# Another order of filler matmuls, search steps and low parts in the routing of a three-stage kernel

## Chip, core and metric

The kernel runs as one program on one core of a Trainium2 chip. A core has five engines with queues of their own: PE (TensorE, matmul), DVE (VectorE), ACT (ScalarE), POOL (GpSimd) and SP, which here only issues DMAs. They run at the same time and wait for each other by semaphores. The metric is the device time of one execution in microseconds (us).

## What is computed

Three stages, one behind the other, all in float32: a linear attention with a decaying state, a dense feed-forward layer, and a layer of 8 experts in which each expert gets exactly 3072 / 8 = 384 rows. Who gets which row is settled in order of the logits: the largest one first, and an expert that is full takes no more.

```python
def _attn_ref(r, k, v, w, u):                  # r, k, v: (4, 8, 768, 48)
    for t in range(S):
        cur = np.einsum('bhd,bhe->bhde', u[None] * kt, vt)
        y[:, :, t] = np.einsum('bhd,bhde->bhe', rt, state + cur)
        state = w[None, :, :, None] * state + np.einsum('bhd,bhe->bhde', kt, vt)

def _moe_ref(x, w_in, w_out, alpha):           # 3072 x 384, 384 x 2048, 2048 x 384
    h = x @ w_in
    g = np.maximum(h, 0.0) + alpha * np.minimum(h, 0.0)
    return g @ w_out

def _moe2_ref(x, w_gate, w1, w2):              # 8 experts, 384 x 1024 and 1024 x 384
    order = np.argsort(-(x @ w_gate).flatten())
    for idx in order:
        tok, e = (int(idx) // E, int(idx) % E)
        if assigned[tok] >= 0 or counts[e] >= cap:
            continue
        assigned[tok] = e
        counts[e] += 1
    for e in range(E):
        mask = assigned == e
        out[mask] = np.maximum(x[mask] @ w1[e], 0.0) @ w2[e]
```

## The kernel before

**Precision.** A float32 product is made of three matmuls of a faster type. Each operand is split in a high part (a copy made on ACT, the names end in `h`) and a low part (the difference, made on DVE or POOL, the names end in `l`), and `product3` adds high x high, high x low and low x high (L1410 to L1412).

**Stages.** Up to about 513 us the kernel computes attention and the first feed-forward layer in six chunks of rows. Then come eight routing rounds and eight experts, overlapped: while PE works for one expert, the search for a later one runs on DVE and PE.

**A routing round** (`route(p)`, L1345) finds which expert fills up next and its 384 rows. It is a search for the value of a logit, in six steps (two levels of three). Step m: DVE compares all keys with 40 marks (`grid`, L1296 or L1298); PE counts the hits for each expert (`count(p, m)`, 12 small matmuls, L1677); DVE turns the counts into hits (`rest`, `hits`, L1303 and L1304); PE adds up which mark was met (`digit(p, m)`, one small matmul, L1712); DVE takes the maximum, the answer (`found`, L1307), and makes the next grid from it. Then `close` (L1309) works out the expert number (`expert`, L1317) and a running sum, PE adds offsets over partitions (`offsets`, L1716), DVE makes slots, `inversion` turns them into matrices `is_a` and `is_b`, PE multiplies these (`inverse`, L1725), and DVE writes the row numbers `idx`. I call the round with p = 0 the first search, p = 1 the second and so on.

**What hangs on a round.** SP waits for the expert number and loads that expert's weights (`raw`, four DMAs of 768 KB, L455 and L457). POOL gathers the 384 rows by `idx` in three gathers (`xg`, L631). PE turns each third of them (`turn_rows`, three transposes, L1736), ACT copies the high part (`rows_hi`, `xeh`, L810), DVE makes the low part (`rows_lo`, `xel`, L1212). From the second expert on all thirds are turned in one PSUM bank, so the turning of third a waits for the low part of third a - 1. ACT and POOL split the weights (`hi`, L797 and L798; `lo`, L641 and L642); POOL also scatters the finished rows (`scatter`, L636).

**The expert stream.** Each expert has 8 hidden groups. `expert_hidden(p, f, k)` is one third of group f, `expert_back(p, f, a)` one third of what it adds to the output; each is one step of three matmuls, 48 steps for an expert. Between them ACT takes the positive part (`relu_hi`, L804) and DVE makes its low part (`relu_lo`, written to `gl`, L1205). The products of `expert_back` with group f wait for the low part of group f.

**What sets the order.** Each engine runs its instructions in the order in which they are written. On PE the function `body(new)` goes through 48 places (`at`); at each it emits what the tables `counts_at`, `digits_at`, `offsets_at`, `inverse_at`, `turns_at` and `busy_at` name, in this order, and then one step of the stream, which lags by 15 places: the first step of the whole stream comes at place 15 of `body(0)`. `body(0)` carries the second search, `body(1)` the third, `body(2)` the fourth; from the fifth on all have the same tables. On DVE the search calls `while_counting(p, m)` between grid and hits and `while_placing(p, m)` between hits and answer; both emit low parts by round and step. `busy(n, bank)` (L1631) emits n filler matmuls of ones, 512 columns each, whose result nobody reads.

The first search ends with `offsets(0)`, `inverse(0, 0)`, `inverse(0, 1)`, and then `body(0)` begins.

## Time and profile before

| | us |
|---|---|
| median of 3 runs | 799.83 |
| lowest and highest of them | 798.2, 801.44 |
| the profiled execution, its time | 800.57 |
| the profiled execution, its span | 798.8 |

| engine | busy us | share of the span |
|---|---|---|
| PE, matmuls | 770.1 | 96% |
| PE, weight loads | 648.8 | 81% |
| DVE | 501.4 | 63% |
| POOL | 473.8 | 59% |
| ACT | 220.7 | 28% |

The chain of work that ended last is 85% PE and 10% DVE. In a timeline row the first number is the start in us from the span's start, the second the duration; then come engine, line, operation, output and inputs by name, and, in brackets, how long the engine was idle before and what ended that. Matmuls are pipelined: the next one starts before the booked duration of the last is over, so it is the distance between starts that counts.

### The profile page before, as it was taken

To read this page: it belongs to the slowest core of one execution; us is meant where nothing else is said; L and a number is where in the kernel's file an instruction comes from. 1 tells how busy PE (TensorE), PEld (TensorE's weight loads), DVE (VectorE), ACT (ScalarE), POOL (GpSimd) and SP (SyncE) were. 2 spreads that over 40 slices of the span, in tenths; PEclk is the share of its full clock that TensorE was granted. 3 is DMA by queue.
4 is the path that set the end of the run, shared out by engine and by line. 5 is a ranking of instruction groups with operands and counts; after the bars stand their busy time and mean duration, and the time that the engine had idled before them with its cause. 6 is when DMAs were issued, how large, how long until landed. Compare 5 with 4: busy or idle time off the path is not lost.

```text
span 798.8 us, 15937 instructions
## 1 busy us (share of the span) xinstructions
PE 770.1 (96%) x6301; PEld 648.8 (81%) x6301; DVE 501.4 (63%) x1047; ACT 220.7 (28%) x453; POOL 473.8 (59%) x469
## 2 busy tenths in 40 slices
PE   6899999999999999999999999978999999999997
PEld 4578888888888888888888788755888989989996
DVE  8887766665655566666654334476877878876221
ACT  1233322111211121112111221204244353353451
POOL 6899985555555555555553332306566775775881
PEclk8999999999999999999999999997999999999999
DMA  8875522222122222221004000015514506417501
GB/s 215 229 203 152 155 71 71 70 57 73 61 61 62 69 70 70 65 69 60 28 11 169 11 31 1 0 55 173 189 59 160 191 29 218 149 70 258 177 14 46
DMA packets 47081, 78.32 MB, mean 98 GB/s; under 512 B 6304, under 2 KB 32032, under 8 KB 46624
## 3 DMA queue, kind: packets, MB, share of 16 engines
q1 hardware_dynamic: 38352, 59.42, 23.3%
q10 hardware_dynamic: 5584, 8.46, 3.8%
q0 software_dynamic: 3072, 9.44, 3.3%
q8 instruction: 50, 0.82, 0.4%
q14 instruction: 23, 0.19, 0.1%
HBM read 67.85 MB, written 9.44 MB: 97 GB/s over the span
## 4 chain that ended last, share of the span: by engine, by line
PE 85%; DVE 10%; issue 2%; POOL 1%; DMA 1%; ACT 1%; POOLq 0%; SPq 0%; DVEq 0%; ACTq 0%
PE bank L1410 24%; PE bank L1412 22%; PE bank L1411 22%; PE bank L1427 3%; PE bank L1461 3%; PE bank L1444 2%; PE bank L1677 2%; PE bank L1520 2%; PE bank L1575 2%; PE bank L1736 1%; DVE both L929 1%; PE bank L1480 1%; DVE grid L1296 1%; POOL gl L539 1%; PE bank L1633 1%
## 5 line engine op out<-in xcount | busy, mean ns | idle before, releaser
L539 POOL TENSOR_TENSOR gl<-g,gh 128x512 fp32r<-128x512 f32 x80 | 107.7, 1346 | 158.1 <-ACT gh L717 158.1
L1072 DVE TENSOR_SCALAR q<-bank,alpha_sb 128x512 f32<-128x512 f32 x96 | 71.9, 749 | 141.1 <-PE bank L1412 140.9
L717 ACT CAST gh<-g 128x512 fp32r<-128x512 f32 x80 | 49.9, 623 | 284.1 <-PE bank L1412 250.9
L1410 PE MATMUL bank<-xTh,win_h 128*128 128x512 f32 x288 | 113.4, 394 | 0.3 <-DVE xTl L965 0.3
L1412 PE MATMUL bank<-xTh,win_l 128*128 128x512 f32 x288 | 112.3, 390 | 0.0
L1411 PE MATMUL bank<-xTl,win_h 128*128 128x512 f32 x288 | 112.2, 390 | 0.0
L1410 PE MATMUL bank<-gh,wout_h 128*128 128x512 f32 x240 | 99.5, 415 | 0.9 <-DVE vs L956 0.3
L1412 PE MATMUL bank<-gh,wout_l 128*128 128x512 f32 x240 | 94.1, 392 | 0.0
L1411 PE MATMUL bank<-gl,wout_h 128*128 128x512 f32 x240 | 93.7, 390 | 0.0
L641 POOL TENSOR_TENSOR w1l<-raw,w1h 128x384 fp32r<-128x384 f32 x64 | 64.8, 1013 | 36.5 <-ACT w2h L798 36.3
L1410 PE MATMUL bank<-xeh,w1h 128*128 128x384 f32 x192 | 69.7, 363 | 0.0
L1410 PE MATMUL bank<-w2h,gh 128*128 128x384 f32 x189 | 66.8, 354 | 0.0
L1410 PEld LDWEIGHTS bank<-xTh,win_h 128*128 128x128 f32 x288 | 54.1, 188 | 15.0 <-issue 2.5
L1412 PE MATMUL bank<-xeh,w1l 128*128 128x384 f32 x192 | 64.8, 338 | 0.0
L642 POOL TENSOR_TENSOR w2l<-raw,w2h 128x384 fp32r<-128x384 f32 x64 | 64.7, 1012 | 0.0
L1411 PE MATMUL bank<-xel,w1h 128*128 128x384 f32 x192 | 64.6, 336 | 0.0
L1412 PE MATMUL bank<-w2h,gl 128*128 128x384 f32 x189 | 63.6, 337 | 0.0
L1411 PE MATMUL bank<-w2l,gh 128*128 128x384 f32 x189 | 63.5, 336 | 0.0
L1412 PEld LDWEIGHTS bank<-xTh,win_l 128*128 128x128 f32 x288 | 54.0, 188 | 11.4
L1411 PEld LDWEIGHTS bank<-xTl,win_h 128*128 128x128 f32 x288 | 54.1, 188 | 10.8
L1081 DVE SCALAR_TENSOR_TENSOR g<-bank,q 128x512 f32<-128x512 f32 x84 | 58.1, 691 | 2.9
L1205 DVE SCALAR_TENSOR_TENSOR gl<-bank,gh 128x384 fp32r<-128x384 f32 x63 | 34.9, 554 | 36.3 <-ACT gh L804 33.4
(239 smaller groups left out, 1584.0 us busy)
## 6 DMA issues: line engine op xcount, KB each, us to landing
raw<-w SPq DMA_DIRECT2D x32, 768.0 KB
rt<-rT SPq DMA_DIRECT2D x48, 96.0 KB, 2.9
vs<-v SPq DMA_DIRECT2D x48, 96.0 KB, 2.9
vn<-v SPq DMA_DIRECT2D x24, 192.0 KB, 2.9
x2rows<-x2n SPq DMA_DIRECT2D x24, 192.0 KB, 1.9
kt<-kT SPq DMA_DIRECT2D x44, 96.0 KB, 2.5
kn<-kN SPq DMA_DIRECT2D x20, 192.0 KB, 2.4
rn<-rN SPq DMA_DIRECT2D x20, 192.0 KB, 2.6
```

Source lines behind the costliest of these rows:

```text
L539: nc.gpsimd.tensor_tensor(gl[:, f % 2], g[:, f % 2], gh[:, f % 2].bitcast(F32), ALU.subtract).then_inc(gl_ready, 1)
L641: nc.gpsimd.tensor_tensor(w1l[:, f], raw1[:, p % 2, :, f * P:(f + 1) * P], w1h[:, f].bitcast(F32), ALU.subtract).then_inc(wlo1_ready, 1)
L642: nc.gpsimd.tensor_tensor(w2l[:, f], raw2[:, p % 2, f, :], w2h[:, f].bitcast(F32), ALU.subtract).then_inc(wlo_ready, 1)
L717: nc.scalar.copy(gh[:, f % 2], g[:, f % 2]).then_inc(gh_ready, 1)
L1072: nc.vector.tensor_scalar(q[:, f % 2], h, 0.0, alpha_sb[:, f:f + 1], ALU.min, ALU.mult).then_inc(q_ready, 1)
L1081: nc.vector.scalar_tensor_tensor(out=g_of(i, f), in0=h, scalar=0.0, in1=q[:, f % 2], op0=ALU.max, op1=ALU.add).then_inc(g_ready, 1)
L1205: V.scalar_tensor_tensor(out=hidden_l(p, f), in0=banks[3 + f % 2][:, 0:CAP], scalar=0.0, in1=hidden_h(p, f).bitcast(F32), op0=ALU.max, op1 ...
L1410: nc.tensor.matmul(o, a_h, b_h, start=first, stop=False)
L1411: nc.tensor.matmul(o, a_h, b_l, start=False, stop=False)
L1412: return nc.tensor.matmul(o, a_l, b_h, start=False, stop=last)
L1427: mm = nc.tensor.matmul(score_bank(c, b, j)[halves(j), h * HT:(h + 1) * HT], kt[heads_in(j), b % 2, h], weights(c, b)[heads_in(j), j, h], ...
L1461: return nc.tensor.matmul(y_bank(c, b)[halves(j), cols], weights(c, b)[:, j, h], vs[:, b, j, cols], start=(h == 0), stop=(h == H - 1), ski ...
```

## The change

Five things, all in the part behind 534 us.

1. Between `offsets(0)` and `body(0)` PE gets 29 fillers in batches, with waits on steps of DVE between them: 4, 3 and 4 ahead of the first half of the inversion, 1 between the halves, 5, 4 and 8 behind it. In `body(0)` the table of fillers goes from 9, 2, 4, 2, 1, 1 to 1, 2, 2, 1, and the turnings from places 2, 4, 4 to 2, 5, 6.
2. Counts and digits of the second, third and fourth search stand at other places, most of them later; offsets and inversion of the second and third search two places later. The turnings of the second expert stand two places earlier.
3. On DVE the low parts that stand between the steps of the second and third search are set to other steps.
4. The expert number is written right behind the maximum that gives it, ahead of the member test, in every round but the last.
5. On POOL the low parts of six weight pieces of the second expert, not four, stand ahead of the first scatter.

```diff
--- before.py
+++ after.py
@@ -647,9 +647,9 @@
             gather(0)
             lo(0, range(NF2))
             gather(1)
-            lo(1, range(NF2 // 2))
+            lo(1, range(NF2 - 2))
             scatter(0)
-            lo(1, range(NF2 // 2, NF2))
+            lo(1, range(NF2 - 2, NF2))
             for p in range(2, E):
                 gather(p)
                 lo(p, range(NF2))
@@ -1251,13 +1251,12 @@
                 if p == 1 and m == 2:
                     rows_lo(0, 0)
                     rows_lo(0, 1)
-                if p == 1 and m == 4:
-                    relu_lo(0, 0)
+                if p == 2 and m == 1:
+                    relu_lo(0, 6)
                 if p == 2 and m == 2:
-                    relu_lo(0, 6)
-                    rows_lo(1, 0)
+                    rows_lo(1, 1)
+                    rows_lo(1, 2)
                 if p == 2 and m == 3:
-                    rows_lo(1, 2)
                     relu_lo(0, 7)
                 if p == 2 and m == 6:
                     relu_lo(1, 1)
@@ -1279,7 +1278,11 @@
                     rows_lo(0, 2)
                 if p == 2 and m == 4:
                     relu_lo(1, 0)
-                if p >= 2 and m == 2:
+                if p == 1 and m == 3:
+                    relu_lo(0, 0)
+                if p == 2 and m == 1:
+                    rows_lo(1, 0)
+                if p >= 3 and m == 2:
                     rows_lo(p - 1, 1)
                 if p == 1 and m >= 5:
                     relu_lo(0, m - 4)
@@ -1310,11 +1313,11 @@
 
                 hold(V.scalar_tensor_tensor(out=full, in0=full_at[1], scalar=found[1], in1=rev1[:], op0=ALU.is_equal, op1=ALU.mult))
                 hold(V.tensor_reduce(fullmax, full, AX_X, ALU.max))
+                V.tensor_scalar(expert[:, p:p + 1], fullmax, -1.0, float(E), ALU.mult, ALU.add).then_inc(expert_ready, 1)
                 hold(V.tensor_scalar(member, rankmax, fullmax, None, ALU.is_equal))
                 step(V.scalar_tensor_tensor(out=sure_tie[:, 0:NT], in0=key2[:], scalar=found[1], in1=member, op0=ALU.is_gt, op1=ALU.mult))
                 hold(V.scalar_tensor_tensor(out=sure_tie[:, NT:2 * NT], in0=key2[:], scalar=found[1], in1=member, op0=ALU.is_equal, op1=ALU.mult))
                 V.tensor_tensor_scan(running[:], ones[:, 0:2 * NT], sure_tie, 0.0, ALU.mult, ALU.add).then_inc(running_ready, 1)
-                V.tensor_scalar(expert[:, p:p + 1], fullmax, -1.0, float(E), ALU.mult, ALU.add).then_inc(expert_ready, 1)
                 hold(V.tensor_scalar(closing, full, fullmax, CLOSED, ALU.is_equal, ALU.mult))
                 hold(V.tensor_tensor(logits[:], logits[:], over_tokens(closing, E), ALU.add))
                 if p >= 2:
@@ -1778,12 +1781,12 @@
             def body(new):
 
                 q = new + 1
-                counts_at = ((2, 5, 18, 23, 27, 31), (7, 11, 15, 19, 23, 27), (3, 7, 12, 17, 21, 25))[new] if new < 3 else (2, 7, 11, 16, 21, 25)
-                digits_at = ((4, 6, 19, 24, 28, 32), (9, 13, 16, 20, 24, 28), (5, 10, 14, 18, 22, 26))[new] if new < 3 else (4, 9, 13, 17, 22, 26)
-                offsets_at = (36, 32)[new] if new < 2 else 30
-                inverse_at = (45, 41)[new] if new < 2 else 39 if new < E - 2 else 26
-                turns_at = ((2, 4, 4), (9, 11, 13), (7, 9, 11))[new] if new < 3 else (5, 7, 10)
-                busy_at = {0: 9, 2: 2, 4: 4, 5: 2, 6: 1, 7: 1} if new == 0 else {}
+                counts_at = ((2, 6, 18, 25, 29, 33), (9, 13, 17, 21, 25, 29), (5, 9, 13, 17, 21, 25))[new] if new < 3 else (2, 7, 11, 16, 21, 25)
+                digits_at = ((4, 7, 22, 26, 30, 34), (11, 15, 18, 22, 26, 30), (7, 11, 14, 18, 22, 26))[new] if new < 3 else (4, 9, 13, 17, 22, 26)
+                offsets_at = (38, 34)[new] if new < 2 else 30
+                inverse_at = (47, 43)[new] if new < 2 else 39 if new < E - 2 else 26
+                turns_at = ((2, 5, 6), (7, 9, 11), (7, 9, 11))[new] if new < 3 else (5, 7, 10)
+                busy_at = {2: 1, 4: 2, 5: 2, 6: 1} if new == 0 else {}
                 for at in range(6 * NF2):
                     if q < E - 1:
                         for m in range(2 * V3):
@@ -1819,8 +1822,19 @@
                 digit(0, m)
                 kept_back(6 if m < 2 * V3 else 3 * B * NF)
             offsets(0)
+            busy(4, banks[3])
+            pe.wait_ge(inv_step, 1)
+            busy(3, banks[3])
+            pe.wait_ge(inv_step, 3)
+            busy(4, banks[3])
             inverse(0, 0)
+            busy(1, banks[3])
             inverse(0, 1)
+            busy(5, banks[3])
+            pe.wait_ge(idx_ready, 2)
+            busy(4, banks[3])
+            pe.wait_ge(onehot_ready, 2)
+            busy(8, banks[3])
             for p in range(E):
                 body(p)
             for s in range(done[0], 6 * NF2 * E - 9):
```

PE, from the end of the first search to the second digit of the second search; `idle_b` is the filler's operand, `is_ar,is_b` the inversion, `id_wg,xg` a turning. Before:

```order
L1725 MATMUL bank<-is_ar,is_b 128x12 x12
L1633 MATMUL bank<-idle_b 128x512 x9
L1677 MATMUL bank<-onehot,grid 128x16 x12
L1736 MATMUL bank<-id_wg,xg 128x128 x3
L1633 MATMUL bank<-idle_b 128x512 x2
L1712 MATMUL bank<-hits,sized 128x8
L1736 MATMUL bank<-id_wg,xg 128x128 x6
L1633 MATMUL bank<-idle_b 128x512 x4
L1677 MATMUL bank<-onehot,grid 128x16 x12
L1633 MATMUL bank<-idle_b 128x512 x2
L1712 MATMUL bank<-hits,sized 128x8
```

and now:

```order
L1636 MATMUL bank<-idle_b 128x512 x11
L1728 MATMUL bank<-is_ar,is_b 128x12 x6
L1636 MATMUL bank<-idle_b 128x512
L1728 MATMUL bank<-is_ar,is_b 128x12 x6
L1636 MATMUL bank<-idle_b 128x512 x17
L1680 MATMUL bank<-onehot,grid 128x16 x12
L1739 MATMUL bank<-id_wg,xg 128x128 x3
L1636 MATMUL bank<-idle_b 128x512
L1715 MATMUL bank<-hits,sized 128x8
L1636 MATMUL bank<-idle_b 128x512 x2
L1739 MATMUL bank<-id_wg,xg 128x128 x3
L1636 MATMUL bank<-idle_b 128x512 x2
```

In the new program count 2, the third turning and digit 2 come behind this piece. The nine fillers behind the inversion are 17, with 12 more ahead; the second and third turning are no longer neighbours.

PE, the first two turnings of the second expert, `body(1)`, before:

```order
L1712 MATMUL bank<-hits,sized 128x8
L1736 MATMUL bank<-id_wg,xg 128x128 x3
L1410 MATMUL bank<-xeh,w1h 128x384
L1411 MATMUL bank<-xel,w1h 128x384
L1412 MATMUL bank<-xeh,w1l 128x384
L1410 MATMUL bank<-xeh,w1h 128x384
L1411 MATMUL bank<-xel,w1h 128x384
L1412 MATMUL bank<-xeh,w1l 128x384
L1677 MATMUL bank<-onehot,grid 128x16 x12
L1736 MATMUL bank<-id_wg,xg 128x128 x3
```

and the second and third of them now:

```order
L1680 MATMUL bank<-onehot,grid 128x16 x12
L1739 MATMUL bank<-id_wg,xg 128x128 x3
L1413 MATMUL bank<-xeh,w1h 128x384
L1414 MATMUL bank<-xel,w1h 128x384
L1415 MATMUL bank<-xeh,w1l 128x384
L1413 MATMUL bank<-xeh,w1h 128x384
L1414 MATMUL bank<-xel,w1h 128x384
L1415 MATMUL bank<-xeh,w1l 128x384
L1715 MATMUL bank<-hits,sized 128x8
L1739 MATMUL bank<-id_wg,xg 128x128 x3
```

Before, the first turning stood behind digit 1 and the second behind count 2; now the second stands behind count 1 and the third behind digit 1.

DVE, the start of the third search (`xel` is the low part of gathered rows, `gl` that of a hidden group), before:

```order
L1296 TENSOR_TENSOR grid<-key,bank 128x24x40
L1303 TENSOR_TENSOR rest<-cap_c,bank 40x8
L1304 TENSOR_TENSOR hits<-bank,rest 40x8
L1307 TENSOR_REDUCE bank<-bank 128x1
L1298 SCALAR_TENSOR_TENSOR grid<-key,bank 128x24x40
L1205 SCALAR_TENSOR_TENSOR gl<-bank,gh 128x384
L1212 TENSOR_TENSOR xel<-bank,xeh 128x3x128
L1303 TENSOR_TENSOR rest<-cap_c,bank 40x8
L1304 TENSOR_TENSOR hits<-bank,rest 40x8
L1212 TENSOR_TENSOR xel<-bank,xeh 128x3x128
L1307 TENSOR_REDUCE bank<-bank 128x1
L1298 SCALAR_TENSOR_TENSOR grid<-key,bank 128x24x40
```

and now:

```order
L1299 TENSOR_TENSOR grid<-key,bank 128x24x40
L1205 SCALAR_TENSOR_TENSOR gl<-bank,gh 128x384
L1306 TENSOR_TENSOR rest<-cap_c,bank 40x8
L1307 TENSOR_TENSOR hits<-bank,rest 40x8
L1212 TENSOR_TENSOR xel<-bank,xeh 128x3x128
L1310 TENSOR_REDUCE bank<-bank 128x1
L1301 SCALAR_TENSOR_TENSOR grid<-key,bank 128x24x40
L1212 TENSOR_TENSOR xel<-bank,xeh 128x3x128 x2
L1306 TENSOR_TENSOR rest<-cap_c,bank 40x8
L1307 TENSOR_TENSOR hits<-bank,rest 40x8
L1310 TENSOR_REDUCE bank<-bank 128x1
```

The low part of the first third of the rows is now made behind the first hits, and those of the second and third stand together behind the second grid.

## Rows read from the trace of the kernel before

**Rows 1.** Windows: length, busy us PE, PEld, DVE, ACT, POOL; then PEclk, DMA, GB/s

```profile
551.00:619.00 68.00, 63.73 (x518) 55.90 (x518) 52.62 (x152) 27.56 (x63) 43.76 (x46) 1.00 0.38 135
660.00:728.00 68.00, 67.59 (x538) 61.74 (x538) 55.30 (x160) 27.62 (x62) 45.89 (x48) 1.00 0.46 160
```

**Rows 2.** The same table, the stretch ahead of the expert stream

```profile
537.00:550.00 13.00, 9.89 (x50) 4.73 (x51) 8.92 (x25) 4.19 (x10) 7.47 (x9) 0.50 0.60 178
```

**Rows 3.** Timeline, PE: start us, us, instruction, idle before and who ended it

```profile
537.97 0.33 PE L1725 MATMUL bank<-is_ar,is_b 128*128 128x12 f16 x6 [2.96 <-DVE is_b L1239]
```

**Rows 4.** Chain that ended last: start us, us, what

```profile
543.17 4.38 DMA xg<-x2rows,idx
```

**Rows 5.** Timeline, all engines, from the third turning to the stream

```profile
547.59 0.90 PE L1736 MATMUL bank<-id_wg,xg 128*128 128x128 f32 x3 [0.38 <-DMA xg<-x2rows,idx]
...
550.82 0.54 DVE L1212 TENSOR_TENSOR xel<-bank,xeh 128x384 fp32r<-128x384 f32 x1
...
551.41 0.44 PE L1410 MATMUL bank<-xeh,w1h 128*128 128x384 f32 x1
```

**Rows 6.** Timeline, turnings of expert 1

```profile
579.58 0.52 PE L1736 MATMUL bank<-id_wg,xg 128*128 128x128 f32 x3 [0.56 <-DVE xel L1212]
...
580.13 0.48 ACT L810 CAST xeh<-bank 128x384 fp32r<-128x384 f32 x1 [2.21 <-PE bank L1736]
...
580.65 0.56 DVE L1212 TENSOR_TENSOR xel<-bank,xeh 128x384 fp32r<-128x384 f32 x1 [0.83 <-ACT xeh L810]
...
581.35 0.52 PE L1736 MATMUL bank<-id_wg,xg 128*128 128x128 f32 x3 [0.18 <-DVE xel L1212]
```

**Rows 7.** Timeline: count, hits, digit, answer, next count of a search step

```profile
553.09 0.46 PE L1677 MATMUL bank<-onehot,grid 128*128 128x16 bf16 x12
...
553.78 0.16 DVE L1304 TENSOR_TENSOR hits<-bank,rest 40x8 bf16<-40x8 f32 x1
...
554.00 0.18 PE L1712 MATMUL bank<-hits,sized 65*128 65x8 bf16 x1 [0.45 <-DVE hits L1304]
...
554.03 0.42 PE L1410 MATMUL bank<-xeh,w1h 128*128 128x384 f32 x1
...
554.21 0.17 DVE L1307 TENSOR_REDUCE bank<-bank 128x1 f32<-128x8 f32 x1 [0.27 <-PE bank L1712]
...
554.64 0.33 PE L1410 MATMUL bank<-xeh,w1h 128*128 128x384 f32 x1
...
555.91 0.46 PE L1677 MATMUL bank<-onehot,grid 128*128 128x16 bf16 x12 [0.59 <-DVE grid L1296]
```

**Rows 8.** Timeline, PE: digit and the next count

```profile
608.01 0.18 PE L1712 MATMUL bank<-hits,sized 65*128 65x8 bf16 x1
...
609.72 0.46 PE L1677 MATMUL bank<-onehot,grid 128*128 128x16 bf16 x12 [0.38 <-DVE grid L1298]
```

**Rows 9.** Timeline, end of the second search and the low parts behind it

```profile
562.60 0.16 DVE L1307 TENSOR_REDUCE bank<-bank 128x1 f32<-128x8 f32 x1
...
566.82 0.55 DVE L1205 SCALAR_TENSOR_TENSOR gl<-bank,gh 128x384 fp32r<-128x384 f32 x1
...
569.39 0.46 PE L1725 MATMUL bank<-is_ar,is_b 128*128 128x12 f16 x12
...
573.64 0.56 DVE L1205 SCALAR_TENSOR_TENSOR gl<-bank,gh 128x384 fp32r<-128x384 f32 x1
```

**Rows 10.** Timeline, PE: two places at which both programs can be compared

```profile
574.53 0.34 PE L1410 MATMUL bank<-w2h,gh 128*128 128x384 f32 x1
...
618.37 0.46 PE L1677 MATMUL bank<-onehot,grid 128*128 128x16 bf16 x12
```

**Rows 11.** Timeline: the expert number and the weight load that waits for it

```profile
564.18 0.13 DVE L1317 TENSOR_SCALAR expert<-bank 128x1 int32<-128x1 f32 x1
...
565.08 0.38 SPq L455 DMA_DIRECT2D raw<-w  x1
```

**Rows 12.** DMA queues, 574 to 575 us, all there are: packets, MB, share

```profile
q1 hardware_dynamic: 242, 0.37, 105.6%
```

## Prediction

> **What bounds the kernel now.** I read the windows table first. From 660 to 728 us, where the experts run in their repeated form, the tensor engine (PE) is busy 67.59 of 68 us; from 551 to 619 us, the part that the tables of the change touch, only 63.73 of 68 [rows 1]. So there are about 4 us of idle PE to win there (a little more, since the ends of matmuls are modelled), and outside it next to nothing. In the first part of the kernel no instruction moves. The second thing to win lies just ahead: from 537 to 550 us the granted clock is 0.50, the lower of its two levels, 1.2 GHz [rows 2]. PE was idle for 2.96 us up to 537.97, then ran fillers at the lower level [rows 3].
>
> **Why the expert stream starts at 551.41.** The third gather lands 4.38 us after 543.17, at 547.55, and the chain of work runs through it [rows 4]. Its turning (three transposes) starts at 547.59 and is booked with 0.90 us; yet the low part of those rows starts only at 550.82, and the stream follows at 551.41 [rows 5]. In between DVE waits for count 2, which stands on PE behind the turning and four fillers at the lower clock.
>
> **Fillers and order at the start.** The change puts 11 fillers ahead of the inversion, one between its halves and 17 behind, each batch tied to a step of DVE, so that PE never idles for long up to the grid of the second search. None of them holds up the inversion by more than 0.1 us: at the full level the 4, 3 and 4 take about 0.2 us each (half of what they take at 1.2 GHz) and fit between the steps of DVE. I take it that the clock stays at 2.4 GHz. Count 2 now stands ahead of the third turning, with one filler behind, so DVE is free when that turning is done. At the full level a turning at 579.58 gives the copy at 580.13 and the low part at 580.65, which lasts 0.56 [rows 6]: 0.55 + 0.52 + 0.56, and 0.04 to PE. The stream starts at 547.6 + 1.7 = **549.3**, a gain of **2.1 us**. The landing itself does not move, since DVE's chain up to the indices is not faster (it is 0.05 us longer by the moved expert number). That the first weights load earlier is worth nothing: the store of the last rows stands ahead of it on SP.
>
> **What a search costs.** All that follows uses one set of steps. Three matmuls of the stream (I call them a step, as the kernel does) take 0.53 us: 551.41 to 553.09 are nine, and the first step behind a small matmul takes 0.61 (554.03 to 554.64). A count allows its digit 0.91 us later (553.09, 554.00); the hits in between end 0.85 after the count. Digit to the answer on DVE 0.21; from there with the change of key to count 4 1.70 us [rows 7]. Elsewhere digit to next count is 1.71 at least, 608.01 to 609.72 [rows 8], so 1.5 from the answer. What DVE does between hits and answer adds to that.
>
> **Second search, step by step.** Count 3 at 549.3 + 1.7 = 551.0; digit 3 now comes behind a step, at 551.95, which hides the wait of 0.6 us that stands between 553.09 and 554.00. But the low part of hidden group 0 now stands between hits 3 and answer 3 and takes 0.55: the answer comes at 552.4, count 4 at 554.1, where PE is ready at 553.6: wait 0.5 (0.75 before). Digit 4 555.1, count 5 556.75, digit 5 557.7. Here PE wants the low part of group 1, which DVE makes only behind hits 5, till 558.15: wait 0.5, new. Count 6 559.8, answer 6 561.2. In the kernel before this answer is at 562.60, the low part of group 3 at 566.82 [rows 9]; 4.2 later is 565.5, done 566.0, where PE wants it at 565.25: wait 0.8, new. The inversion on PE stands two steps later than before, at 568.65; the low part of group 5 starts 4.25 behind it (569.39 to 573.64), after the indices and the next front [rows 9], so 568.65 + 4.25 + 0.55 = 573.5. PE wants it at 572.7: wait 0.8, new. The product that needs it starts at 573.5, against 574.53 before [rows 10]. **Half of the 2.1 us is gone; 1.0 is left**, because the stream now runs ahead of DVE and waits for it.
>
> **Third search: the turnings.** The gathers of expert 1 are turned at places 7, 9, 11 and no longer at 9, 11, 13, while counts and digits move back by two. Turning 0 meets its landing, about 574.4: wait 0.4. The load of expert weights ahead of it starts 2.2 us earlier: expert number to load takes 0.9 (564.18 to 565.08) [rows 11], and the number itself comes 0.9 sooner in a chain that is 1.3 sooner. In the trace, between 574 and 575 us the queue of the weights holds all engines at 105.6% and the gather, issued at 570.78, has no packet [rows 12]. The Trainium skill, page DMA: Bandwidth & Descriptors, section on queues, rings and completion order, says that an engine goes round between the queues that have work; by that the earlier load would do nothing for turning 0, by the row it does, and the sum differs by less than 0.3 us. The row decides.
>
> Turning 1 follows count 1 at once (575.9). It may start only when the low part of rows 0 is made, and that now stands behind hits 1: 575.9 + 0.85 + 0.55 + 0.14 (from 581.21 to 581.35, [rows 6]) = 577.4, so PE waits **1.2 us**. Turning 2 follows digit 1 at once (578.8) and needs the low part of rows 1, which stands behind the grid of count 2: 578.8 + 0.21 + 0.21 + 1.14 + 0.55 + 0.14 = 581.1, a wait of **2.2 us**. Before, the waits at these two turnings were 0.56 and 0.18 as booked, about 1.0 with their handovers. The low part of rows 2 comes behind the copy of hidden group 7, which is done only after turning 2: two ACT operations of 0.5 with their handovers, so 583.1 to 583.7; digit 2 at 584.1, and the stream of expert 1 behind it. The rest by the same steps: waits of 0.5, 0.2 and 0.3 at counts 3, 4, 5, digit 6 at 595.05, offsets 597.3, inversion 602.1 to 602.6. The later places of these give back 0.3 of what the turnings cost.
>
> **Fourth search.** Its counts 1 to 3 and digits 1 and 2 stand two or one places later; count 3 used to let the low part of group 6 be ready in time, now PE reaches its product a wait of 0.95 earlier than DVE. Count 4 stands at the same place as before (17) and comes at **619.0 against 618.37** [rows 10]. From there both programs are alike and PE bound, and the shift stays: +0.6. The expert number ahead of the member test adds 0.05 us to each later chain: +0.1 in all.
>
> **Other edits.** The low parts of six instead of four weight pieces ahead of the first scatter: POOL has the same work, it idled there for the scatter's rows, and the pieces are wanted over 5 us later: 0. If POOL were the late one, 1 us for each piece.
>
> **Sum.** -2.1 + 1.0 or so (waits behind DVE in the second search) + 1.7 (third, net) + 0 to 0.1 (fourth) + 0.1 = **+0.8 us**. The profiled execution has a span of 798.8 and a time of 800.57; the median is 799.83. I put the sum on the median: **800.6**. Bounds of the unknown handovers: 0.1 us at each of some 15, so 1.5 either way.
>
> **Rivals.** (1) *The lead is kept.* If the low parts reach PE in time (DVE is quicker through the third search than I step it), the 1.0 us lead at 573.5 stays and the old waits in 575 to 619 go too, of which [rows 1] allows about 3: 796 to 799. For it: each count and digit does get more room. Against: the turnings stand behind DVE work in program order; a quicker DVE can't change that. Chance 0.15. (2) *Slower: the clock falls again.* From 543.1, when the 17 fillers end, to 549.3 PE has work for under two thirds of the time: turnings, counts and eight fillers. The lower level was granted after an idle stretch that was only 3 us long [rows 3], and it held for 13 us although PE was busy 9.89 of them [rows 2]. If it falls here, the start goes back by up to 2.0 and the first 3 to 6 us of the stream take nearly twice as long, 1.5 to 3 more: 804 to 805.6. It decides as soon as the level is low at 549. Chance 0.12. (3) *The fillers do not lift the clock at all*, so that only the order counts: the start gains 1.5, the rest as in my sum: 801.5. Chance 0.03. My forecast: 0.70.
>
> **Numbers.** Forecast 800.6, range 797.0 to 804.0 (most of rival 1 and the near edge of rival 2, with the bounds of the handovers). Half a per cent, 4 us, is about what a measurement of this kernel can tell from no change. Faster by more: 0.05 (the far end of rival 1). Slower by more: 0.12. The same: 0.83.
>
> **What would show it.** Right: clock 1.00 from 530 on without a break; stream start near 549.3; PE waits for DVE's low parts at the turnings of expert 1 near 577 (over 1 us) and 579 to 581 (about 2 us); count 4 of the fourth search near 619. Wrong: the turnings wait under 0.5 us each (rival 1), or a clock of 0.50 in any row from 543 to 555 (rival 2). My sum would be wrong too if the stream's start moved by much less than 2 us at a full clock, which would mean that the landing of the gather moved.

## The result and the profile after

The changed kernel takes 802.18 us (median of 20 runs, 800.23 to 803.48), the kernel before 800.19 beside it (20 runs, 798.07 to 801.55). The ratio is 1.0021, with an interval of 1.0012 to 1.003: slower, by an amount that stays within half a per cent. The forecast was 800.6 with a rise of 0.8 us; the rise is 1.7 by the ratio and 2.0 by the medians. The profiled execution took 800.81, with a span of 799.1. Two executions of the kernel before, 1237.59 and 1237.78 us at a mean granted clock of 0.56, were taken beside the experiments and stand in no ratio and no spread below.

Windows of the changed kernel, columns as in [rows 1] and [rows 2]:

```profile
537.00:550.00 13.00, 10.07 (x80) 5.02 (x79) 10.42 (x29) 4.44 (x11) 7.83 (x9) 1.00 0.68 221
551.00:619.00 68.00, 61.66 (x505) 53.91 (x504) 50.46 (x148) 27.38 (x63) 43.71 (x46) 1.00 0.37 127
660.00:728.00 68.00, 67.58 (x539) 61.71 (x538) 55.29 (x160) 27.54 (x62) 45.83 (x48) 1.00 0.47 161
```

The clock of the first stretch is 1.00 where [rows 2] had 0.50. But between 551 and 619 PE is busy for 61.66 us, 2.1 less than in [rows 1]: what the start won was lost there. The repeated form from 660 on is the same.

The timeline of the changed kernel at the start of the expert stream answers [rows 5]:

```profile
538.88 4.26 PE L1636 MATMUL bank<-idle_b 128*128 128x512 bf16 x17
...
547.60 0.53 PE L1739 MATMUL bank<-id_wg,xg 128*128 128x128 f32 x3
...
548.68 0.56 DVE L1212 TENSOR_TENSOR xel<-bank,xeh 128x384 fp32r<-128x384 f32 x1
...
549.29 0.45 PE L1413 MATMUL bank<-xeh,w1h 128*128 128x384 f32 x1 [0.50 <-DVE xel L1212]
```

From turning to low part it is 1.08 us, not 3.23, and the stream starts at 549.29. What leads to it is not what led to it before. The chain that ended last runs here through the first gather:

```profile
540.31 4.63 DMA xg<-x2rows,idx
...
546.01 1.23 DVE grid L1301
...
547.29 0.46 PE bank L1680 x12
547.75 0.39 PE bank L1739 x3
```

The third gather, issued at 543.04, lands after 3.1 us, at about 546.1, and nobody waits for it; the third turning stands behind count 2, and count 2 waits for the grid of DVE. In the kernel before, the third gather took 4.38 us and was what PE waited for [rows 4].

The turnings of the second expert, the answer to [rows 6], PE and DVE:

```profile
574.30 0.55 PE L1739 MATMUL bank<-id_wg,xg 128*128 128x128 f32 x3 [0.21 <-DMA xg<-x2rows,idx]
...
575.73 0.46 PE L1680 MATMUL bank<-onehot,grid 128*128 128x16 bf16 x12
...
577.20 0.52 PE L1739 MATMUL bank<-id_wg,xg 128*128 128x128 f32 x3 [1.01 <-DVE xel L1212]
...
578.61 0.18 PE L1715 MATMUL bank<-hits,sized 65*128 65x8 bf16 x1
...
580.87 0.52 PE L1739 MATMUL bank<-id_wg,xg 128*128 128x128 f32 x3 [2.08 <-DVE xel L1212]
```

```profile
576.43 0.16 DVE L1307 TENSOR_TENSOR hits<-bank,rest 40x8 bf16<-40x8 f32 x1
576.51 0.54 DVE L1212 TENSOR_TENSOR xel<-bank,xeh 128x384 fp32r<-128x384 f32 x1
...
579.04 1.22 DVE L1301 SCALAR_TENSOR_TENSOR grid<-key,bank 128x960 bf16<-128x960 f32 x1
580.18 0.55 DVE L1212 TENSOR_TENSOR xel<-bank,xeh 128x384 fp32r<-128x384 f32 x1
```

Read the two together. Turning 1 stands right behind count 1 on PE; the low part that it waits for stands behind the hits of that same count on DVE. Turning 2 stands behind digit 1; its low part stands behind the answer and the whole next grid. PE waits 1.01 and 2.08 us. The list of PE's waits from 530 us to the end says the same in one place (engine, line, waited for: us in total, times, longest):

```profile
PE bank L1739 <- DVE xel L1212: 3.7, 5, 2.1
PE bank L1413 <- DVE gl L1205: 2.1, 4, 0.8
PE bank L1739 <- DMA xg<-x2rows,idx: 1.0, 2, 0.8
```

**A yardstick for all kernels.** From count 4 of the fourth search on, every kernel of this study is alike: the time of the profiled execution less the start of that count is 182.13 to 182.22 us in all thirteen. So two distances in the trace, with the time at which the first inversion starts, tell the whole story: from the first half of the first inversion to the stream's start (A), and from there to that count (B).

| kernel | A | B | profiled | median | ratio to before, interval |
|---|---|---|---|---|---|
| before | 13.44 | 66.96 | 800.57 | 800.19 | |
| changed | 11.43 | 69.34 | 800.81 | 802.18 | 1.0021 (1.0012 to 1.003) |
| changed, again | 11.53 | 70.54 | 802.61 | 802.26 | 1.0027 (1.0015 to 1.0038) |
| start alone | 11.44 | 66.00 | 797.75 | 797.73 | 0.9971 (0.9962 to 0.9979) |
| turnings back | 11.35 | 66.44 | 797.22 | 797.82 | 0.9979 (0.9965 to 0.9993) |
| expert number alone | 12.19 | 66.05 | 798.13 | 800.37 | 1.0002 (0.9989 to 1.0014) |
| no paced fillers | 12.45 | 70.38 | 802.5 | 802.49 | 1.0033 (1.002 to 1.0046) |
| search part alone | 13.21 | 71.37 | 804.02 | 803.37 | 1.0037 (1.0025 to 1.0049) |
| five edits | 11.55 | 66.57 | 797.79 | 798.13 | 0.9973 (0.9962 to 0.9985) |
| fillers in the waits | 11.43 | 69.34 | 800.79 | 801.27 | 1.0008 (1.0 to 1.0017) |
| low parts of rows earlier | 11.42 | 66.22 | 797.96 | 798.1 | 0.9977 (0.9967 to 0.9988) |
| order at start alone | 12.64 | 67.49 | 800.62 | 799.15 | 1.0001 (0.9986 to 1.0016) |
| best try | 11.49 | 65.79 | 796.67 | 797.05 | 0.9965 (0.9953 to 0.9977) |

The first inversion itself starts at 537.26 to 538.37 in these executions: about 1.1 us of spread come from ahead of the change. Four kernels (no paced fillers, search part alone, five edits, fillers in the waits) ran on another chip than the other experiments. The kernel before had a median of 800.37 beside them, and 800.11 and 800.01 beside the others; the changed kernel, unaltered, was not among the experiments there. Between the two chips the ratios are the safer measure.

### The profile page after: what moved, and what is told of

Its sections match the earlier page's. It is cut to its first block, busy times and chain, and to the rows that moved or that the text cites. A ratio compares the mean times of both kernels' runs of the same rounds, so it can differ in the third digit from the quotient of the medians.

```text
span 799.1 us, 15969 instructions
## 1 busy us (share of the span) xinstructions
PE 769.1 (96%) x6317; PEld 647.4 (81%) x6317; DVE 501.2 (63%) x1047; ACT 219.9 (28%) x453; POOL 473.6 (59%) x469
## 4 chain that ended last, share of the span: by engine, by line
PE 83%; DVE 10%; POOL 2%; issue 2%; DMA 1%; ACT 1%; POOLq 0%; SPq 0%; DVEq 0%; ACTq 0%
PE bank L1413 23%; PE bank L1415 22%; PE bank L1414 22%; PE bank L1430 3%; PE bank L1464 3%; PE bank L1447 2%; PE bank L1523 2%; PE bank L1680 2%; PE bank L1578 2%; DMA xg<-x2rows,idx 1%; PE bank L1739 1%; POOL gl L539 1%; DVE both L929 1%; DVE grid L1299 1%; DVE grid L1301 1%
```

## The experiments

**The changed kernel again, unaltered.**

> The changed kernel itself, unaltered, as the common measure on this chip. By every theory its span lies 0.3 to 2 us above the kernel before. The rival in which the clock falls in the sparse stretch between 543 and 549 us says more: its executions split in two groups about 2 us apart, and the group with the longer time has the lower mean granted clock (0.989 to 0.992 against 0.993 to 0.999); a low level would show in the profile between 543 and 560 if the profiled execution belongs to it. Without that rival the times form one group.

802.26 (800.12 to 803.33), about 2 us above the kernel before once more, so the change is dearer than my sum of 0.8. The single times of all 32 runs of the changed kernel fall into two groups, 11 from 800.1 to 800.9 and 21 from 801.6 to 803.5. This profile came from the second group, the first one from the first. The stream starts 0.61 us later in the second, at 549.90, and is still 0.5 us later at count 1 of the third search (576.23 against 575.73); it has the same two waits. Then, in windows of 1 us (columns as in [rows 1]), the second profile has

```profile
580.00:581.00 1.00, 0.00 (x0) 0.00 (x0) 1.00 (x2) 0.00 (x0) 0.00 (x0) 1.00 0.00 0
581.00:582.00 1.00, 0.64 (x4) 0.67 (x4) 0.22 (x1) 0.00 (x0) 0.00 (x0) 0.70 0.00 0
582.00:583.00 1.00, 1.00 (x6) 1.00 (x5) 0.00 (x0) 0.00 (x0) 0.00 (x0) 0.50 0.00 0
583.00:584.00 1.00, 1.00 (x5) 0.69 (x4) 0.00 (x0) 0.79 (x3) 0.00 (x0) 0.50 0.00 0
584.00:585.00 1.00, 1.00 (x16) 1.00 (x16) 0.83 (x3) 1.00 (x4) 0.03 (x1) 0.59 0.00 0
585.00:586.00 1.00, 1.00 (x8) 0.84 (x7) 0.14 (x2) 0.72 (x2) 1.00 (x2) 1.00 0.00 0
```

and the first profile has 1.00 in all of them. Right behind the two waits the granted clock falls to 0.50, 1.2 GHz, for about 3.4 us; matmuls of the stream start 0.32 us apart instead of 0.17. B is 70.54 instead of 69.34: **the waits cost a second time, 1.2 us**. The groups came as the expectation says, but the clock falls here and not between 543 and 549. The mean granted clock of an execution goes with its group only loosely: 19 of the 21 in the upper group have 0.989 to 0.993, the other two 0.997 and 0.999; the lower group has 0.991 to 0.999. So how often the clock falls is an estimate from the times.

**The start alone.** The kernel before with the fillers between `offsets(0)` and `body(0)` and these lines:

```diff
-counts_at = ((2, 5, 18, 23, 27, 31), ...
-digits_at = ((4, 6, 19, 24, 28, 32), ...
-turns_at = ((2, 4, 4), ...
-busy_at = {0: 9, 2: 2, 4: 4, 5: 2, 6: 1, 7: 1}
+counts_at = ((2, 6, 18, 23, 27, 31), ...
+digits_at = ((4, 7, 19, 24, 28, 32), ...
+turns_at = ((2, 5, 6), ...
+busy_at = {2: 1, 4: 2, 5: 2, 6: 1}
```

> The kernel before with the start of the changed one alone: the 29 fillers, and of the second search the first two counts and digits, the turnings and the fillers at places 2 to 7. Everything from place 8 on is as before. My theory: the stream starts at 549.3 as in the changed kernel, the turnings of expert 1 keep their old places and their short waits (under 0.6 us each), so part of the 2.1 us stays: 1 to 1.8 us below the kernel before, 2 to 3 below the changed one. The rival that the lead cannot be kept because DVE holds the stream in the second search, whatever stands behind, gives 0 to 0.5 below the kernel before.

797.73, 4.5 us below the changed kernel, and 2.4 below the kernel before, where 1 to 1.8 was expected. The start is worth 2.4 by the medians (1.7 to 3.0 by the interval), and it makes the time steady: 797.05 to 798.59, where the kernel before spreads over 3.5 to 5 us.

**The turnings back at their places.** The changed kernel with one edit:

```diff
-turns_at = ((2, 5, 6), (7, 9, 11), (7, 9, 11))
+turns_at = ((2, 5, 6), (9, 11, 13), (7, 9, 11))
```

> The changed kernel with one triple put back: the turnings of expert 1 at places 9, 11, 13 again. My theory charges the turnings at 7, 9, 11 with waits of 1.2 and 2.2 us; at 9, 11, 13 I step waits of 0.6 and 0.15, and 0.6 at digit 2: about 2 us below the changed kernel, and 0.5 to 1.5 below the kernel before. The rival that DVE is simply late in the third search, and PE waits for it in another place when the turnings do not, gives less than 0.5 us.

797.82, more than was expected: 4.4 below the changed kernel. PE's wait for `xel` falls from 3.7 us to 0.8; that for `gl` stays, that for `hits` rises from 0.3 to 0.8:

```profile
PE bank L1413 <- DVE gl L1205: 2.1, 4, 0.8
PE bank L1739 <- DVE xel L1212: 0.8, 4, 0.3
PE bank L1715 <- DVE hits L1307: 0.8, 2, 0.5
```

B falls by 2.9 us against the changed kernel's first profile (66.44 against 69.34), all at full clock, and in most executions there are the 1.2 us of the clock besides: that one tuple of places is nearly the whole loss. Of the other edits to the searches, B shows 0.4 us (66.44 against 66.00 in the start alone).

**The expert number alone.** The kernel before with the `expert` line ahead of `member`.

> The kernel before with the expert number alone written ahead of the member test. My theory: 0.05 us more on each chain to the indices, none of it awaited for long, and a weight load 0.6 to 0.9 us earlier that nobody waits for: within 0.3 us of the kernel before. The rival that the weight load is what holds the stream somewhere (ACT does wait for it at 572) would give a gain of 0.5 us or more.

800.37 against 800.11: nothing, as expected.

**No paced fillers.** The changed kernel without the 29 fillers and the waits between them.

> The changed kernel without its 29 paced fillers ahead of body(0); the tables, the DVE order and the rest as in the changed kernel. My theory: without them PE idles about 3 us ahead of the inversion, the granted clock is 0.50 from about 537 on, and with only eight fillers left in body(0) nothing lifts it before the expert stream: counts, turnings and the first matmuls of the stream run at half pace. Expert stream starts 0.5 to 1 us later than in the changed kernel (its 549.3), and the stream's first microseconds are slow, 1 to 3 us more: 803.5 to 806 in all, 1.5 to 4 above the changed kernel. Rival (the order at the start brings the gain, the fillers nothing, my rival 3 in the prediction): stream start within 0.3 us of the changed kernel's plus 0.6, time within 0.8 of the changed kernel, 801.5 to 803.

802.49, within 0.3 of the changed kernel by the medians, and 0.5 to 1.0 us above it by the ratios (1.0033 against 1.0027 and 1.0021): the rival's number for the time. The clock was low from about 538, but it was back by 549; in the last 6 us PE was busy for 5.21. Windows of this kernel:

```profile
543.00:549.00 6.00, 5.21 (x41) 3.43 (x41) 3.34 (x9) 2.89 (x7) 4.49 (x5) 0.55 0.27 72
549.00:553.00 4.00, 3.06 (x28) 2.74 (x28) 2.71 (x7) 2.44 (x6) 2.80 (x3) 1.00 0.92 334
```

A is 12.45 against 11.43, so with the fillers the stream starts 1.0 us earlier. My expectation that the stream's first microseconds would be slow as well was wrong for this execution. One profile and intervals over 1 us wide can't settle whether the medians, too, differ by 1.0. The clock fell behind the turnings here too (B 70.38).

**The search part alone.** The changed kernel with the start of the kernel before.

> The changed kernel with the start of the kernel before: no paced fillers, and in body(0) the places up to 7 for counts, digits, turnings and fillers are those of before. So the later places of the searches, the earlier turnings of the second expert, the DVE order, the expert number and the POOL part stand alone. If the two parts add up, this is the kernel before (800.1) plus what separates the changed kernel from the one with the start alone (802.3 - 797.7 = 4.5): 804 to 805, and the stream starts at 551.4, two waits of about 1.0 and 2.1 us at the turnings near 579 and 583. If the waits depend on the lead of 2 us that the new start brings (a later stream gives DVE more time), the waits at the products behind low parts, 2.1 us in all, shrink and the time is 801.5 to 803.

803.37, ratio 1.0037. The second case, under which the waits would shrink, is wrong, since PE waits for `gl` for the same 2.1 us and for `xel` 3.8. Full addition would be 1.0056 (1.0027 - 0.9971). That lies above the interval of 1.0025 to 1.0049, but as a difference of two measured ratios it is itself known only to about 0.0014 either way, so it isn't shown that the parts fail to add up. In the profiled executions they nearly do: A + B is 84.58 here and 80.40 in the kernel before, 4.2 more, and 82.07 and 77.44 in the changed kernel's second profile and the start alone, 4.6 more.

A is not one number without the fillers: 13.44, 13.21 and 12.19 in the kernel before, here, and in the expert number alone, which have the same start. Two things differ. The clock between 543 and 549 is 0.50, 0.97 and 0.75. And the third gather lands 4.4, 4.9 and 3.1 us after its issue. In the kernel before it still has a packet after 546.9, and PE waits for the landing. Over all thirteen profiles the third gather takes 3.0 to 3.2 us in each of the eight with paced fillers, and 4.4, 4.9, 4.9, 4.4 and 3.1 in the five without. Whether the fillers have to do with that, and what the late packets wait for, no run here shows.

**Five edits.** Turnings back; low parts of groups 1 and 2 ahead of the hits; inversion at 45; low part of group 5 ahead of the keys; fourth search as before.

```diff
                 front_rank(slice(0, NT))
+                if p == 1:
+                    relu_lo(0, 5)
...
-                if p == 1:
-                    relu_lo(0, 5)
```

> The changed kernel with five edits: turnings of the second expert at places 9, 11, 13; the low parts of hidden groups 1 and 2 between grid and hits of the second search, not behind the hits; inversion of the second search at place 45, not 47; the low part of group 5 right behind the front's ranks; counts and digits of the fourth search at the places of before. It is to beat both kernels. Waits at products behind low parts of hidden groups (2.1 us in the changed kernel, 4 times) should fall to under 1, and the time to 795.5 to 797, 0.8 to 2 below the kernel with the turnings back alone (797.8). If those waits lie off the bound (what is won there is lost again at the next step that waits for the search), it is 797.3 to 798.3, no better.

798.13, no better. The waits for `gl` did fall, from 2.1 to 0.5 us, but others took their place (first lines of PE's waits):

```profile
PE bank L1680 <- DVE grid L1299: 1.8, 3, 1.0
PE bank L1680 <- DVE grid L1301: 1.2, 4, 0.4
```

One I made myself. The low part of group 5 now stands at a point where ACT has not yet written its high part, and the keys of the third search wait behind it on DVE:

```profile
570.29 0.56 DVE L1205 SCALAR_TENSOR_TENSOR gl<-bank,gh 128x384 fp32r<-128x384 f32 x1 [1.09 <-ACT gh L804]
```

From the inversion to the next count 1 it is 7.05 us here and 6.00 in the start alone.

**Fillers in the two waits.** The changed kernel with work of no use where PE idles:

```diff
                         if at == turns_at[a]:
+                            if new == 1 and a > 0:
+                                pe.wait_ge(g2l_ready, 7)
+                                busy(4 if a == 1 else 9, banks[3])
                             turn_rows(new, a)
```

> The changed kernel with fillers in the two waits that its earlier turnings make: 4 ahead of the second turning of the second expert, 9 ahead of the third, behind a wait on the low part of hidden group 6. They fill idle time and do nothing else, so the stream loses the same 1.2 and 2.2 us to DVE. Theory (in most executions the clock falls behind these two waits and that costs 1.2 us or more on top of the idle time): the slow group of times, 801.6 to 803.5, goes, all executions stand at 800.2 to 801, median 800.5, and the profile has a clock of 1.00 in every window from 575 to 590. Rival (the two groups of times have another cause, and the clock in these windows does not matter): median 802 to 802.6 as in the changed kernel, or 0.1 to 0.4 above it, spread as before.

801.27, 1.0 below the changed kernel by the medians and 1.0 to 1.5 by the ratios, and the upper group is gone: the highest of 11 runs is 801.73. The median is 0.8 above what was expected; the spread left, 1.7 us, is close to the 1.5 of the start alone. The turning comes where it came before, and the clock holds:

```profile
578.63 2.10 PE L1636 MATMUL bank<-idle_b 128*128 128x512 bf16 x9
580.85 0.41 PE L1739 MATMUL bank<-id_wg,xg 128*128 128x128 f32 x2
```

```profile
581.00:586.00 5.00, 4.70 (x47) 3.94 (x47) 2.74 (x6) 2.51 (x6) 2.30 (x3) 1.00 0.00 0
```

B is 69.34, to the hundredth that of the changed kernel's first profile. So idle time and clock are told apart: against the start alone the stream loses 3.3 us at full clock (69.34 - 66.00), 2.9 of it at the turnings, and about 1.2 more to the clock in two executions of three, going by the groups of times.

**Low parts of rows one step earlier.** Turnings still at 7, 9, 11; only DVE's order differs:

```diff
                 if p == 2 and m == 1:
-                    relu_lo(0, 6)
+                    rows_lo(1, 0)
                 if p == 2 and m == 2:
-                    rows_lo(1, 1)
                     rows_lo(1, 2)
...
                 if p == 2 and m == 1:
-                    rows_lo(1, 0)
+                    relu_lo(0, 6)
+                    rows_lo(1, 1)
```

> The changed kernel, turnings of the second expert still at places 7, 9, 11, but with the low parts of its rows one step earlier on DVE: rows 0 behind the first grid of the third search (ahead of the hits, where the low part of hidden group 6 stood), group 6 and rows 1 behind the hits, rows 2 behind the second grid. If the two long waits come from where DVE makes these low parts (my prediction's step), and not from the earlier places as such or from the gather's landing, the wait at turning 1 falls from 1.0 to about 0.3 us, at turning 2 from 2.1 to about 0.3, count 2 of the third search comes 2.5 us earlier, no clock below 1.00 in 575 to 590, and the time is that of the kernel with the turnings back, 797.2 to 798.5. If the earlier turnings as such are too early, the waits move to the copies on ACT or to the counts and the time stays above 800.

798.1, as expected. Turning 1 starts without a wait of note, turning 2 after 0.18:

```profile
576.30 0.52 PE L1739 MATMUL bank<-id_wg,xg 128*128 128x128 f32 x3
...
578.08 0.52 PE L1739 MATMUL bank<-id_wg,xg 128*128 128x128 f32 x3 [0.18 <-DVE xel L1212]
```

The earlier places were not wrong in themselves; the order on DVE did not go with them.

**The order at the start alone.** The four lines of the start alone, without the fillers ahead of the inversion and behind it.

> The kernel before with the start's order alone: count 2 of the second search at place 6 ahead of the third turning, turnings at 2, 5, 6, digit at 7, fillers 1, 2, 2, 1 in body(0), and no paced fillers. With the start in full the time was 797.7; the changed kernel without its paced fillers was at most 0.7 us slower than with them. If the order carries the gain (rival 3 of the prediction: 1.5 of 2.1), the stream starts near 550.0 and the time is 798 to 799. If the fillers carry it, 799.5 to 801. In either case the spread of the single times should be wider than with the fillers (1.5 us from lowest to highest there, 5 in the kernel before), since the clock falls and rises at its own time ahead of the stream.

799.15 against 800.01, ratio 1.0001 (0.9986 to 1.0016): not to be told from no change, and between the two cases of the expectation; single times from 798.41 to 803.75. In its profile A is 12.64, 0.8 less than before, but the clock stays low into the stream (0.50 from 549 to 553 too) and B is 1.5 longer than in the start alone. Half of the gain of the start, or more, goes with the fillers.

**The best try.** The kernel of the low parts of rows, and for the second search: low parts of groups 1 and 2 ahead of the hits, that of group 3 at the end of `close`, inversion at 45.

> The kernel of the low parts of rows one step earlier, and for the second search: low parts of hidden groups 1 and 2 between grid and hits, that of group 3 behind the close of the search and not behind is_a, inversion at place 45. It leaves the low part of group 5 where it is (the kernel that moved it ahead of the keys had 1.1 us of DVE waiting for ACT there). Waits at products behind low parts of hidden groups fall from 2.1 to 0.8 to 1.3 us in total. If the search chain is shortened with it, 796.3 to 797.4, the fastest of all; if what is won there is lost at the grid of the next search, as in the kernel with five edits, 797.3 to 798.3.

797.05 (796.67 to 797.83), the lowest time of the study. It beats both kernels of this case; that it beats the start alone the intervals don't show. Here DVE is ahead, and turning 0 meets the gather:

```profile
573.24 0.55 PE L1741 MATMUL bank<-id_wg,xg 128*128 128x128 f32 x3 [1.18 <-DMA xg<-x2rows,idx]
```

## Why the forecast was right, and where its sum was off

**The start: the number right, the path to it not.** 549.3 was forecast, 549.29 came, with the clock at 1.00 throughout. The gain is 2.1 us by the stream's start, 2.0 by A, 2.4 between medians of the start alone. But the prediction let the landing of the third gather stay at 547.55 and hang the third turning on it. It landed at about 546.1. The turning came at 547.60 all the same, since it stands behind count 2, and count 2 stands behind DVE's grid; that chain comes from the first gather, which landed at 544.94. That the two paths meet within 0.1 us is luck. The gather's 4.38 us in the kernel before would have made a landing at 547.42 here and moved nothing. I also had the parts of the gain wrong: rival 3 gave 1.5 us to the order alone, which measured 0.8 in A and nothing safe in the median.

**Second search: right in kind.** The waits behind low parts of groups 1, 3 and 5 were forecast at 0.5, 0.8, 0.8 and came at 0.26, 0.50, 0.60; the product that waits last starts at 573.29 (forecast 573.5, before 574.53 [rows 10]).

**Third search: right, place by place.** Turning 0 waits 0.21 (0.4 was forecast); turning 1 at 577.20 (577.4), turning 2 at 580.87 (581.1), digit 2 at 583.86 (584.1), digit 6 at 594.72 (595.05), inversion at 601.86 (602.1).

**Fourth search.** The wait for group 6 is 0.76 (0.95), count 4 at 618.63 (619.0). So in the first profile every step stands within 0.4 us, and the shift against [rows 10] is 0.26. That profile is of the smaller group; its agreement with the forecast (800.81 against 800.6) is closer than that of the median, 802.18.

**What the sum missed: 1.2 us.** It priced the waits at the turnings as idle time only. My rival 2 had the mechanism, a clock that falls behind partly idle PE, but at another place (543 to 549, where PE was busy 3.81 of 6 us and the clock held), and I did not ask the same of my own forecast of 576 to 581, where I had PE wait for 3.4 us of 5. In the first profile PE is busy for 1.72 of the 4 us from 577:

```profile
577.00:581.00 4.00, 1.72 (x11) 1.54 (x12) 1.91 (x4) 0.48 (x1) 0.20 (x1) 1.00 0.01 2
```

The Trainium skill, page TensorE: Matmul & The Clock Gate, Part 1 on the HAM clock gate, says that the chip looks at PE's activity in windows that run free of the program, so that one kernel meets them at different phases. By that the clock may fall behind a stretch like this in some executions and not in others. The two profiles of the changed kernel fit that (0.50 in one, 1.00 in the other); neither shows such a window.

**What the sum missed: the reference.** The search part costs 3.3 us of B at full clock (69.34 - 66.00); I had 2.7 (from 549.3 to 619.0 it is 69.7, against 66.96). The 66.96 is too long: the profiled execution of the kernel before holds a late handover from PE to DVE that none of the three other kernels with this order shows. Its count 6 of the third search starts at 591.31, and DVE gets it only at 592.79:

```profile
591.31 0.46 PE L1677 MATMUL bank<-onehot,grid 128*128 128x16 bf16 x12
...
592.79 0.17 DVE L1303 TENSOR_TENSOR rest<-cap_c,bank 40x8 f32<-40x8 f32 x1 [1.06 <-PE bank L1677]
...
593.20 0.18 PE L1712 MATMUL bank<-hits,sized 65*128 65x8 bf16 x1 [0.80 <-DVE hits L1304]
```

In the start alone the same pair is 0.50 us apart, not 1.48:

```profile
589.48 0.46 PE L1677 MATMUL bank<-onehot,grid 128*128 128x16 bf16 x12
...
589.98 0.17 DVE L1303 TENSOR_TENSOR rest<-cap_c,bank 40x8 f32<-40x8 f32 x1
```

PE itself went on: the next product starts at 591.63, as early behind the count as elsewhere, and only the digit waits, 0.80 us, for the hits that DVE made late. I took the 618.37 of [rows 10] as the kernel's, and with it 0.95 us of chance: count 6 of this search to count 1 of the next is 15.27 us here and 14.31 to 14.32 in the three others. Why DVE got this count late the trace doesn't say.

**The sum as measured:** -2.4 (start, between medians) + 3.3 (the order of the searches, 2.9 of it at the turnings; from profiles) + 1.2 (the clock behind them, in two executions of three) + 0 (expert number) = +2.1, against 1.7 to 2.0 between the kernels. My rival 1 (the lead is kept) fell at the point named against it: the turnings stand behind DVE's work in program order. With that order mended, its 796 to 799 is where four kernels land.

**Open.** The two groups of the changed kernel are some 2 us apart, the clock accounts for 1.2; in the second profile the first inversion also came 0.5 us later, but whether that goes with the group isn't known.

## What to carry to other kernels

Where a table moves an instruction on one engine, look up on the other engine what stands ahead of the thing that it waits for; two steps earlier on PE are worth nothing if DVE makes the operand behind the next grid. Price a wait on PE twice: as idle time, and as a clock that may fall behind it; here it fell behind two waits of 1 and 2 us with work between them. Where a forecast of one instruction comes true, look at what it waited for as well: the number can be right by another path. And before one execution serves as the yardstick, compare its stretches with a second one: here 1 us of it was chance, in a late handover.

## What the runs showed of the hardware

**The second expert's gather starts as the weight load runs out.** Queue q1 carries the weights, q0 the gathers; packets, MB and share by windows of the changed kernel, 571 to 572 us, then 572 to 573, then 573 to 574:

```profile
q1 hardware_dynamic: 244, 0.37, 105.7%
...
q1 hardware_dynamic: 184, 0.26, 75.7%
q0 software_dynamic: 37, 0.14, 39.5%
...
q0 software_dynamic: 87, 0.25, 68.2%
q1 hardware_dynamic: 6, 0.00, 1.5%
```

The gather was issued at 569.83 and had no packet up to 572. In the best try it was issued 2.2 us earlier and landed only 1.06 us earlier, again as q1 ran out. The row of [rows 12] was no exception. It isn't only the time that a gather needs to get going: the last expert's gather, issued at 753.00 with q1 empty, has its first packets in the window from 754.50 to 754.75, 1.5 us or a little more behind the issue, where the one behind the weight load has its first after 572.25, 2.4 us behind the issue, and in the best try over 3 us behind it. For this gather the taking of turns between queues that the prediction weighed does not show. Elsewhere in the same trace it does: from 695.99 to 696.24 q0 and q1 have 25 packets each. What makes the difference isn't known.

**The clock can fall without one long pause.** Behind 1.01 us of idle time, 1.4 of work and 2.08 of idle time the granted clock stayed at 1.00 in one profile of the changed kernel and fell to 0.50 in the other. It fell behind the same waits in the profiles of the kernel without paced fillers (0.50 from 583 to 586) and of the search part alone (0.50 from 583 to 586). In the changed kernel the fall lasted about 3.4 us, although PE was busy for nearly all of it. Without the paced fillers the distance A alone ranges from 12.19 to 13.44, with them from 11.35 to 11.55.
